# Experts stage: where VectorE stands with the uses of a step, in their own step or behind the scores of the next

## What is computed

```python
for e in range(E):                      # E = 4, B = 4, S = 576, D = 512, Hd = 64
    q = x @ wq[e]; k = x @ wk[e]; v = x @ wv[e]
    scores = scale * (q @ k.transpose(0, 2, 1))
    scores = np.where(causal, -1e9, scores)
    scores = scores - scores.max(-1, keepdims=True)
    a = np.exp(scores)
    a /= a.sum(-1, keepdims=True) + 1e-09
    ye = a @ v @ wo[e]
    out += mask_e * w_e * ye            # the two best gates of a token
# then h = U, V mixing over tokens: u = x + (x^T U V)^T
```

## Time and profile before

| | us |
|---|---|
| median of 3 runs | 1225.81 |
| lowest and highest run | 1225.3 and 1225.85 |
| the profiled execution's own time | 1227.07 |
| its span, first to last instruction | 1225.3 |
| mean granted TensorE clock | 0.982 of full speed |

### The profile page before, as it was taken

How to read it: one execution, slowest core, us unless ns; L and a number is a source line. 1 busy time by engine, 2 the same in 40 slices (tenths; PEclk the granted TensorE clock), 3 DMA queues, 4 the chain that set the end, 5 groups by cost and what they waited for, 6 DMA issues and landing times. The chain is left out here.

```text
span 1225.3 us, 19538 instructions
## 1 busy us (share of the span) xinstructions
PE 1151.2 (94%) x7232; PEld 959.4 (78%) x7232; DVE 661.9 (54%) x1497; ACT 541.3 (44%) x1131; POOL 507.1 (41%) x482
## 2 busy tenths in 40 slices
PE   6999999999999999978898989869999999999998
PEld 4777777777777777767777777559898989899896
DVE  4777887877778778836556666465121211112120
ACT  4666666556666666535555656434020211111010
POOL 5788899998888888643222222110000000000000
PEclk9999999999999999989999999979999999999999
DMA  8111112222111111030000001115010101010000
GB/s 199 53 53 51 54 56 59 59 59 59 58 56 53 52 53 35 20 137 1 1 2 36 5 24 42 40 57 145 19 33 1 52 1 51 0 51 0 26 1 26
DMA packets 47559, 54.56 MB, mean 45 GB/s; under 512 B 10992, under 2 KB 29424, under 8 KB 46960
## 3 DMA queue, kind: packets, MB, share of 16 engines
q1 hardware_dynamic: 47472, 53.42, 14.5%
HBM read 43.97 MB, written 9.44 MB: 44 GB/s over the span
## 5 line engine op out<-in xcount | busy, mean ns | idle before, releaser
L545 DVE TENSOR_REDUCE part_max<-psA 128x1 f32<-128x384 f32 x480 | 258.9, 557 | 76.6 <-PE psA L331 56.7
L496 ACT ACTIVATE pT<-psA 128x576 f32<-128x576 f32 x288 | 187.3, 652 | 168.5 <-PE psA L350 161.2
L249 POOL TENSOR_TENSOR pT<-pT 128x576 f32<-128x576 f32 x160 | 229.1, 1432 | 27.3 <-ACT pT L496 6.8
L331 PE MATMUL psA<-kT,qT 128*128 128x384 f32 x480 | 182.1, 393 | 12.5 <-DVE part_max L545 8.2
L364 PE MATMUL psA<-pT,v_raw 128*64 128x288 f32 x1152 | 153.9, 412 | 0.0
L341 PE MATMUL psA<-qT,kT 128*128 128x288 f32 x576 | 133.3, 313 | 0.4 <-ACT pT L496 0.4
L1577 ACT ACTIVATE hid_hi<-psC 128x384 fp32r<-128x384 f32 x96 | 47.0, 489 | 190.4 <-PE psC L1489 190.4
L331 PEld LDWEIGHTS psA<-kT,qT 128*128 128x128 f32 x480 | 90.0, 193 | 46.8 <-DVE part_max L545 30.4
L350 PE MATMUL psA<-qTm,kT 128*128 128x288 f32 x576 | 123.8, 297 | 0.2 <-ACT qTm L482 0.2
L1601 DVE SCALAR_TENSOR_TENSOR hid_lo<-psC,hid_hi 128x384 fp32r<-128x384 f32 x96 | 53.5, 557 | 127.7 <-ACT hid_hi L1577 127.7
L364 PEld LDWEIGHTS psA<-pT,v_raw 128*64 128x64 f32 x1152 | 77.1, 137 | 53.2 <-issue 6.7
(11 more groups left out here) (158 smaller groups left out, 1933.7 us busy)
## 6 DMA issues: line engine op xcount, KB each, us to landing
k_raw<-in_k SPq DMA_DIRECT2D x32, 288.0 KB, 3.0
v_raw<-in_v SPq DMA_DIRECT2D x32, 288.0 KB, 2.8
q_raw<-in_q SPq DMA_DIRECT2D x32, 256.0 KB, 3.3
w_raw<-in_moe_w_ch SPq DMA_DIRECT2D x1, 4096.0 KB, 12.4
u_rows<-x_all SPq DMA_DIRECT2D x16, 256.0 KB, 2.0
w_raw<-in_moe_w_ch SPq DMA_DIRECT2D x16, 256.0 KB, 2.7
u_first<-u_rows SPq DMA_DIRECT2D x3, 768.0 KB, 4.5
u_second<-u_rows SPq DMA_DIRECT2D x3, 768.0 KB, 4.8
```

The costliest lines, as they stand in the source:

```text
L249: nc.gpsimd.tensor_tensor(pT[:, KT, :], pT[:, KT, :], pT[:, j, :], ALU.add).then_inc(part_summed, 1)
L331: nc.tensor.matmul(maxes[n % 2][:, 0:PIECE], qT[h % 3][:, t * P:(t + 1) * P], kT[u][:, c * PIECE:(c + 1) * PIECE], start=True, stop=True). ...
L496: nc.scalar.activation(pT[:, j, :].rearrange("p (a c) -> p a c", a=2), scores[n % 2][:, :, 0:HALF], ACT.Exp, scale=0.5 * float(D) ** -0.5) ...
L545: nc.vector.tensor_reduce(part_max[u][:, t, c:c + 1], maxes[n % 2][:, 0:PIECE], AX.X, ALU.max).then_inc(max_freed[n % 2], 1)
```

## The change

`AT_ONCE` goes. On VectorE all uses of a step but the last are now dealt with in the step itself, in front of the next step's maximum; only the last use of a step waits behind that maximum. The other engines call `over_segments` without `late` and keep their order.

```diff
     LAG = 3
-    AT_ONCE = ("down",)
...
                         uses = [(of_batch(s, u), u)
                                 for u in step_uses(e, i, s == 0, s == batches - 1)]
-                        waiting = [bu for bu in uses if late and bu[1][0] not in AT_ONCE]
-                        for b, use in uses:
-                            if (b, use) not in waiting:
-                                do(b, use)
+                        at_once = len(uses) - 1 if late else len(uses)
+                        for b, use in uses[:at_once]:
+                            do(b, use)
+                        waiting = uses[at_once:]
```

## The result

The changed kernel takes 1238.93 us (median of 4 runs, 1236.93 to 1239.9), the kernel before 1225.83 beside it: a ratio of 1.0103 (95% interval 1.0091 to 1.0115), 13.1 us slower. The forecast was 5.3 us slower with a range up to 1238. The direction was right, the size was not. Two executions of experiments further down (1592.09 and 2765.48 us, where the others of the same kernels took 1227 to 1238) are left out of the medians. The profiled execution took 1239.48 us, its span 1237.7 (12.4 more than before), at a mean granted clock of 0.974 instead of 0.982.

What follows compares the result with a forecast made beforehand. TensorE bounds the experts stage; late maxima would reach it through a VectorE-ScalarE loop. Terms 1.9 - 0.15 + 1.15 - 0.6 + 1.15 + 0.5 + 1.3 = +5.25 us on 1225.81 give 1231.1 us; 8-in-10 range 1221 to 1238.

Steps and rivals of the forecast that it cites:

- new ones of the kinds named: TensorE would wait for `xT_lo` at the pv of (2,4) and first vg, and longer for `moe_pT` at (0,3).
- The loop: Maximum, exponential, high part, low part, next maximum, through VectorE and ScalarE: 3.1 us a step, 3.0 for narrow first tiles.
- the x steps: Steps (2,2) to (2,4): late maxima delay the first vg, +1.15 us each in the second and third batch.
- The first batch: No `down`, wo or u there, so TensorE has less per step; first vg about 1.9 us later.
- The turn of a batch: Steps (3,2) to (0,3): vg's bank sooner -0.7, gates +1.05, loop +0.15; taken as -0.15, -0.6 and +0.5 us.
- the last batch: No x there, but the score of (2,4) waits for the late exponential of (2,2): +1.3 us.
- the wait ahead of the pv of (0,3): TensorE's wait for `moe_pT` at the turn of a batch would grow from about 1 to 2.5 us.
- a rival of 0.15: Longer TensorE waits drop two to five more groups to the lower clock, 1.45 us each: +3 to +7, about 1236; 0.15.
- Wrong if the new waits sum to less than the 13 us that go: Test of the forecast: TensorE's new waits must reach the 13 us of waits for VectorE's low parts that go.
- No change: Rival: shorter loop, each batch loses only what vg gives back, the turn's +1.05 hides; about +1, 1226.8 us; chance 0.13.
- Faster: Rival: late maxima never reach TensorE and its waits just go; 1212.8 us at most, 1219 if half stays; chance 0.17.
- are freed in time, under VectorE's idle time: The qk of (3,2) and (3,3): vg gets its bank 0.73 us sooner, u 1.75; only the first is kept.

Runs made afterwards that it cites:

- the turn alone: The changed kernel with the new rule kept only at expert 0's steps and `down`, other steps waiting behind the next maximum: 1238.34 us, ratio 1.0094.
- The gates: The changed kernel with the five instructions that finish the gates put back behind the maximum of (0,1): 1235.0 us (median of 5), ratio 1.0068.

## Why the prediction was wrong in size

**What held.** The waits of TensorE for `moe_kT` went, and new ones of the kinds named came. VectorE's maxima in the second batch, as in the earlier trace rows (the copy that masks, in front of the maximum of (2,0), (2,1), (2,2), (2,3) and (2,4)):

```profile
641.11 0.28 DVE L1324 COPY_PREDICATED psB<-later,minus 128x128 f32<-128x128 int32 x1
...
643.80 0.28 DVE L1324 COPY_PREDICATED psB<-later,minus 128x128 f32<-128x128 int32 x1
...
647.09 0.30 DVE L1324 COPY_PREDICATED psB<-later,minus 128x128 f32<-128x128 int32 x1
...
650.45 0.29 DVE L1324 COPY_PREDICATED psB<-later,minus 128x128 f32<-128x128 int32 x1
...
654.07 0.21 DVE L1324 COPY_PREDICATED psB<-later,minus 64x64 f32<-64x64 int32 x1
```

TensorE is 4.26 us behind as the stretch begins. Against that they come 1.5, 2.0, 0.6, 2.0 and 1.9 us later; the forecast was 1.4, 2.2, 1.0, 2.4 and 2.4. The loop from (2,0) to (2,1) is 2.69 us, where the forecast took 3.0 for narrow tiles: the rows from which it came stand at a turn, where ScalarE has more in front of a high part. This is why the x steps cost 0.63 and 0.60 us and not 1.15 each: the term had the right mechanism and was sized from another place. ScalarE's row of `down` moved likewise, from 640.19 to 645.05, 0.6 us against TensorE's steps and not 1.0:

```profile
645.05 0.59 ACT L39 ACTIVATE mixed<-psB 128x512 fp32r<-128x512 f32 x1
```

The first batch cost 2.34 (forecast 1.9); the last 0.1 (1.3): the score of (2,4) waits 1.18 us instead of 0.59, and `p` behind gives the same amount back, which the forecast left out.

**The turn of a batch.** The forecast counted +1.05 for the five gate instructions and let the first two turns hide it. From the maximum of (3,4) to that of (0,1) in the fourth batch VectorE took 6.38 us before (728.52 to 734.90) and takes 8.29 now: +1.91. VectorE and GpSimd in one list:

```profile
735.34 0.22 DVE L1324 COPY_PREDICATED psB<-later,minus 64x64 f32<-64x64 int32 x1 [0.21 <-PE psB L1038]
...
736.77 0.83 POOL L974 TENSOR_SCALAR moe_probs<-moe_probs,moe_sum_inv,gate 128x512 f32<-128x512 f32 x1 [2.06 <-DVE moe_sum_inv L1317]
...
737.08 0.62 DVE L1285 TENSOR_TENSOR beats<-beats,before_m 128x80 f32<-128x80 f32 x1
...
740.84 0.82 POOL L974 TENSOR_SCALAR moe_probs<-moe_probs,moe_sum_inv,gate 64x576 f32<-64x576 f32 x1 [3.23 <-DVE moe_sum_inv L1317]
741.18 0.51 DVE L1300 SCALAR_TENSOR_TENSOR gate<-rank,gate 128x20 f32<-128x20 f32 x1
...
741.87 0.42 POOL L989 CAST moe_kT<-moe_kT 64x288 fp32r<-64x288 f32 x1 [0.22 <-ACT moe_kT L39]
741.93 0.39 DVE L1303 TENSOR_SCALAR gate_sum<-gate_sum 128x5 f32<-128x5 f32 x1
...
743.63 0.28 DVE L1324 COPY_PREDICATED psB<-later,minus 128x128 f32<-128x128 int32 x1
```

Three of VectorE's instructions end at 737.70, 741.69 and 742.32, right behind the ends of GpSimd's at 737.60, 741.66 and 742.29. In the trace of before the same three found GpSimd idle; the first gate instruction took 0.16 us, and the other two:

```profile
731.07 0.24 DVE L1286 TENSOR_TENSOR beats<-beats,before_m 128x80 f32<-128x80 f32 x1
...
736.41 0.17 DVE L1304 TENSOR_SCALAR gate_sum<-gate_sum 128x5 f32<-128x5 f32 x1
```

That is 0.38 + 0.35 + 0.22 = 0.95 us, and with the 1.05 forecast it makes the 1.91 within 0.1. The Trainium skill, SBUF — State Buffer, SBUF: two separate sides, says that VectorE and GpSimd share a pair of ports which one of them holds for a whole instruction, and that this concerns a VectorE instruction in a mode that uses both ports, or one with two inputs in SBUF when GpSimd's reads SBUF. The rows agree for the first two (two inputs). The third has one input; no row shows in which mode it ran. That moving these rows by a microsecond would set them against GpSimd is the step that the forecast lacked. The other two turns have the same stretched rows (0.51 to 0.63, 0.39 and 0.62 us). On TensorE the turns came out at +0.77, -0.19 and +0.85 (forecast -0.15, -0.6, +0.5). Without the 1.25 that the clock gave back at the second of them it is +0.77, +1.06 and +0.85, about 2.9 us more than forecast, as much as three times 0.95. The x steps and the last batch, 2.3 us smaller than forecast, made up for most of it, and the clock's 1.25 us for the rest. The sum of 5.1 is right by luck: errors cancel in it, and a gain of the clock is among them.

**The clock is the step that failed.** The forecast wrote that the wait ahead of the pv of (0,3) would grow from about 1 to 2.5 us, had a row in which the same products ran slowly behind a wait of 1.20 us, and still put the lower clock aside as a rival of 0.15. The wait grew to 3.1, and at all three turns and the end of the last batch TensorE ran at the lower clock: 8.2 us by the rows. Filling the wait at two of the turns made the kernel 6.75 us faster. The clock wasn't a case beside the forecast; it belonged in its sum. "Behind the long wait" holds for the turns to the third and fourth batch. At the turn to the second it was low before the long wait, among shorter ones of 0.93, 0.24 and 0.72 us. The rival's price was nearly right as well (two to five groups at 1.45; it was four, at 1.15 to 2.44), and 5.25 + 7.25, its upper end, would have been within a microsecond of the result. "Wrong if the new waits sum to less than the 13 us that go" was the right test for the sign: 16.5 came and 11.0 of the 13.0 went.

**The other rivals.** *No change* is refuted by the 13.1 us. *Faster* is refuted for the change as it is: the pv of (2,4) started 0.5 us late against TensorE's steps, not early. It is right for one part of it, the qk of (3,2) and (3,3): -7.1 us alone, some 2.7 of it by the clock. The forecast had seen that these "are freed in time, under VectorE's idle time", but reckoned that only 0.7 of it would be kept. In the changed kernel that was so, since the turn behind took it all back.

**What stays open.** Which of the turn's uses carries how much was not taken apart beyond the gates; the kernel with the turn alone loses 11.9 us, the one with the qk of experts 2 and 3 alone 3.3, the two share (0,4), and no sum of the parts was found to give 13.1 closely. Why the clock also falls at 784 to 796 in the changed kernel, where no wait is longer than 0.91 us, was not found; it stayed at 1.00 there when two of the turns were filled. Filling the turn to the second batch was not tried. What decides whether a wait of 1 to 2 us is followed by a slow group was not found either: it differs between kernels, and within one kernel from execution to execution.

## What to carry to other kernels

When an in-order engine is given work sooner, look first at whether anyone waits for that work: two uses of each batch had a waiter in front of an idle VectorE, and doing only those gained 7 us where doing all lost 13. A wait on the engine that binds has two prices, its own length and what the clock does around it, so a forecast that lets a wait grow where the trace already shows a slow group must carry the clock in its sum. And a loop through two engines is to be sized from rows at its own place, with the third engine's rows beside them.

## What the runs showed of the hardware

- Behind a wait of 2.8 to 3.1 us twenty products of 128x288 took 4.00 us, three times, and 2.12 at the full clock. There is no clear line in the wait just ahead of them: 1.01, 1.32, 1.33 and 1.69 us were followed by 2.12, but 1.20, 1.57 and 1.95 by 3.57, 3.49 and 3.57, and with no wait ahead such a group took 3.59 (645.63, above). Products without use in the wait kept the clock at 1.00 at both turns that had them. The kernel was 6.75 us faster with them. The Trainium skill, TensorE: Matmul & The Clock Gate, What's actually happening, has the slow state as the default that activity releases; these runs agree in that products in the wait kept the clock up.
- Executions of one kernel, with "The gates" put back, took 1230.92 to 1238.34 us at mean granted clocks of 0.982 to 0.973, the slower the lower.
- Some of VectorE's short instructions beside one of GpSimd took 0.39 to 0.62 us instead of 0.16 to 0.24 and ended 0.02 to 0.10 us behind its end, while a TENSOR_REDUCE passed beside one in 0.18.
